# A gated recurrence with two expert stages: solve levels cut to the triangle's nonzero columns, own part's matmuls among level 3's

## The reference

```python
for t in range(S):
    y[:, :, t] = np.einsum('bhd,bhde->bhe', rt, state)
    Sa = np.einsum('bhde,bhe->bhd', state, at)
    state_decay = state * wt[:, :, None, :] - np.einsum('bhd,bhe->bhde', Sa, bt)
    state = state_decay + np.einsum('bhd,bhe->bhde', vt, kt)
```

## Time and profile before

| | |
|---|---|
| median of 3 runs | 992.5 us (991.58 to 993.65) |
| profiled execution | 993.9 us, span 992.2 us |
| TensorE busy | 947.2 us, 95% of the span |
| VectorE, ScalarE, GpSimd busy | 465.9, 270.5, 275.8 us |
| recurrence | about the first 385 us of the span |
| L956 (levels 2 and 3), L958 (level 4), L1028 (own) | 3072, 1536 and 1536 matmuls; 54.5, 18.1 and 20.7 us busy |

### The profile page before, as it was taken

How to read it: one execution, slowest core, us unless ns; L and a number is a source line. 1 busy time by engine, 2 the same in 40 slices (tenths; PEclk the granted TensorE clock), 3 DMA queues, 4 the chain that set the end, 5 groups by cost and what they waited for, 6 DMA issues and landing times.

```text
span 992.2 us, 51897 instructions
## 1 busy us (share of the span) xinstructions
PE 947.2 (95%) x23581; PEld 732.5 (74%) x23582; DVE 465.9 (47%) x964; ACT 270.5 (27%) x503; POOL 275.8 (28%) x297
## 2 busy tenths in 40 slices
PE   4689999999999999999999999999999999999995
PEld 3579989899898996454554554557888888888884
DVE  5447877887887762423143143162352322222220
ACT  1224444444444442201202202202212122122120
POOL 4535566556656651000011010010052101111111
PEclk9789999999999999999999999999999999999999
DMA  5216442333333321780100100047421111001000
GB/s 147 64 50 209 140 123 89 114 104 119 96 115 111 89 72 41 238 271 0 38 27 24 42 28 20 1 133 256 130 88 61 34 34 39 23 28 33 27 29 3
DMA packets 57704, 81.63 MB, mean 82 GB/s; under 512 B 22274, under 2 KB 37454, under 8 KB 57648
## 3 DMA queue, kind: packets, MB, share of 16 engines
q1 hardware_dynamic: 33536, 58.87, 19.0%
q10 hardware_dynamic: 21088, 13.32, 5.2%
q0 software_dynamic: 3024, 8.72, 2.4%
HBM read 68.04 MB, written 14.45 MB: 83 GB/s over the span
## 4 chain that ended last, share of the span: by engine, by line
PE 91%; issue 3%; DVE 2%; DMA 2%; POOL 1%; ACTq 0%; ACT 0%; POOLq 0%; SPq 0%; DVEq 0%
PE ps_D L1478 14%; PE ps_D L224 12%; PE ps_G L1460 6%; PE ps_E L1460 6%; PE ps_B L236 5%; PE ps_E L956 5%; PE ps_B L188 3%; PE ps_G L1467 3%; PE ps_D L1039 3%; PE ps_A L930 3%; PE ps_G L188 3%; PE ps_D L990 2%; PE ps_E L954 2%; PE ps_E L188 2%; PE ps_D L930 2%
## 5 line engine op out<-in xcount | busy, mean ns | idle before, releaser
L1478 PE MATMUL ps_D<-room,hT 128*128 x496 | 139.1, 433 | 0.8 <-issue 0.8
L224 PE MATMUL ps_D<-room 128*128 128x384 f32 x384 | 126.7, 489 | 0.6 <-DVE room L291 0.6
L1478 PEld LDWEIGHTS ps_D<-room,hT 128*128 128x128 f32 x496 | 91.8, 190 | 35.9 <-issue 1.3
L224 PEld LDWEIGHTS ps_D<-room 128*128 128x128 f32 x384 | 72.1, 190 | 51.5 <-issue 1.6
L1421 POOL DMA_INDIRECT out<-y,token x31 | 35.6, 1147 | 258.3 <-DVE y L1585 224.7
L550 POOL DMA_INDIRECT sorted_rows<-rows,slot x24 | 23.9, 997 | 278.3 <-DVE slot L542 272.2
L894 POOL TENSOR_TENSOR room<-room 32x256 f32<-32x256 f32 x96 | 69.5, 724 | 106.5 <-DVE room L1310 101.1
L1521 ACT ACTIVATE hT<-ps_G 128x512 f32<-128x512 f32 x31 | 18.5, 598 | 217.6 <-PE ps_E L1467 211.4
L1585 DVE TENSOR_SCALAR y<-ps_D,x_in 128x320 f32<-128x320 f32 x31 | 17.0, 550 | 125.9 <-PE ps_D L1478 117.5
L1568 DVE COPY w_own<-room 128x1024 f32 x62 | 44.9, 729 | 62.3 <-PE ps_G L1460 33.8
L291 DVE TENSOR_TENSOR room<-ps_D,room 128x384 f32<-128x384 f32 x32 | 17.8, 558 | 113.2 <-PE ps_D L224 107.8
(11 more groups left out here) (225 smaller groups left out, 1646.2 us busy)
## 6 DMA issues: line engine op xcount, KB each, us to landing
room<-in_moe_w SPq DMA_DIRECT2D x8, 1280.0 KB, 12.6
room<-in_moe_w SPq DMA_DIRECT2D x8, 1024.0 KB, 9.2
room<-in_kb SPq DMA_DIRECT2D x48, 160.0 KB
room<-in_vt SPq DMA_DIRECT2D x24, 320.0 KB, 3.1
x_in<-sorted_rows ACTq DMA_DIRECT2D x27, 161.0 KB, 2.3
room<-in_w SPq DMA_DIRECT2D x48, 82.7 KB
room<-in_a SPq DMA_DIRECT2D x48, 80.0 KB
room<-in_r SPq DMA_DIRECT2D x48, 80.0 KB
```

The source lines that it names most:

```text
L224: mm = pe.matmul(self.vs_bank[n % 2][:, 0:TH], self.v[:, s, d * P:(d + 1) * P], self.wspT[:, s, t * TH:(t + 1) * TH], start=(s == 0), stop ...
L1478: mm = pe.matmul(self.ps_y, side.hT[:, u % 2, f, :], self.weights.w2[:, bass.ds(e, 1), f, :], start=(f == 0), stop=(f == self.NF - 1))
```

## The change

- Levels 2, 3 and 4 take as moving operand only the columns from 4, 8 and 16 on (`NONZERO`), in both halves; so 56, 48 and 16 columns instead of 64, 64 and 32. Squares and sums copy and add these columns alone.
- The powers of levels 2 and 3 get a buffer each beside the sum (`powers`, with `sums` as its last part), whose columns below `NONZERO` are set to zero once, by two small memsets at the start.
- `solveT` gets its first 16 columns by a copy on ScalarE from the sum after level 3, for which `unknowns` has a new wait (`solve_d`).
- own_part is no longer a group of its own between level 2 and scores_r. Its 64 matmuls are issued one by one behind each of the 64 of level 3 (`level_and_own`).
- ScalarE does square 3 ahead of the drain of `own`, then the new copy.

```diff
--- before.py
+++ after.py
@@ -658,13 +658,14 @@
         eng.wait_ge(self.blank_tile, 16)
 
 
-ZEROED = 13
+ZEROED = 15
 CONSTANTS = 29
 CH = 32
 CHUNKS = SEQ // CH
 GROUPS = 16
 WCOLS = GROUPS * (CH + 1) + 1
 ROUNDS = 5
+NONZERO = (0, 0, 4, 8, 16)
 Counts = namedtuple("Counts", "fixed now after later now2 after4 after16 now32")
 
 
@@ -683,7 +684,9 @@
         kb_end = sb("kb_end", 8, 2, 2, CH)
         kb_next, kb_tok = sb("kb_next", 2, 8, 2, HALF), sb("kb_tok", 8, 2, HALF)
         xa, xf = sb("xa", 2, 4, 2, CH), sb("xf", 2, 4, 2, CH)
-        pw, qi, qs = sb("pw", 8, CH), sb("qi", 2, 8, CH), sb("qs", 2, 8, CH)
+        pw, qi = sb("pw", 8, CH), sb("qi", 2, 8, CH)
+        powers = sb("powers", ROUNDS - 1, 8, CH)
+        sums = powers[:, ROUNDS - 2]
         solveT = sb("solveT", 8, CH)
         own, rhs = sb("own", 4, 2, HD), sb("rhs", 4, 2, HD)
         vu, vu_d = sb("vu", 2, 4, 2, HALF), sb("vu_d", 8, 2, HALF)
@@ -721,7 +724,7 @@
         q_d = [sem(f"q{n}_drained") for n in range(ROUNDS - 1)]
         flip_d = [sem(f"flip{n}_drained") for n in range(ROUNDS - 1)]
         sum_d = [sem(f"sum{n}_drained") for n in range(ROUNDS)]
-        xa_d, xf_d, init_d = (sem(x) for x in ("xa_d", "xf_d", "init_d"))
+        xa_d, xf_d, init_d, solve_d = (sem(x) for x in ("xa_d", "xf_d", "init_d", "solve_d"))
         scan_f, scan_b, whole_d, inv_d = (sem(x) for x in ("scan_f", "scan_b", "whole_d", "inv_d"))
         grow_d, ae_d, kbe_d, faded_d = (sem(x) for x in ("grow_d", "a_end_d", "kb_end_d", "faded_d"))
         passed = sem("waits_passed")
@@ -934,7 +937,7 @@
                     pe.wait_ge(y_d, t.after)
                     turn(B, lambda m: faded[:, m].rearrange("p n e -> p (n e)"), fT_f)
 
-                def doubling(t, l):
+                def level(t, l, own=False):
                     if l == 0:
                         pe.wait_ge(xf_d, t.later)
                         if not t.fixed or t.after >= 1:
@@ -946,6 +949,7 @@
                         else:
                             pe.wait_ge(sum_d[l - 1], t.after)
                     pe.sem_inc(passed, 1)
+                    kept = slice(NONZERO[l], CH)
                     for j, n, mp, o in blocks():
                         q, i = quad(2 * mp + o), 2 * n + j
                         if l == 0:
@@ -953,14 +957,28 @@
                         elif l == 1:
                             mm = pe.matmul(E[q, :, i, :], pw[q, i, :], qi[q, :, i, :], start=True, stop=True)
                         elif l < ROUNDS - 1:
-                            mm = pe.matmul(E[q, :, i, :], pw[q, i, :], qs[q, :, i, :], start=True, stop=True)
+                            mm = pe.matmul(E[q, :, i, kept], pw[q, i, :], powers[q, l - 2:ROUNDS - 1:ROUNDS - l, i, kept],
+                                           start=True, stop=True)
                         else:
-                            mm = pe.matmul(E[q, 1, i, :], pw[q, i, :], qs[q, 1, i, :], start=True, stop=True)
+                            mm = pe.matmul(E[q, 1, i, kept], pw[q, i, :], sums[q, i, kept], start=True, stop=True)
+                        if own:
+                            k = quad(2 * mp + 1 - o)
+                            last = pe.matmul(G[q, i * HD:(i + 1) * HD], xa[k, o, n, j, :], v_tok[k, o, n, j, :],
+                                             start=True, stop=True)
                     mm.then_inc(round_f[l], 1)
+                    if own:
+                        last.then_inc(own_f, 1)
+
+                def level_and_own(t, l):
+                    pe.wait_ge(ld_v, t.after16)
+                    if not t.fixed or t.now >= 1:
+                        pe.wait_ge(own_d, t.now)
+                    level(t, l, own=True)
 
                 def unknowns(t):
                     pe.wait_ge(rhs_d, t.now)
                     pe.wait_ge(sum_d[4], t.now)
+                    pe.wait_ge(solve_d, t.now)
                     pe.sem_inc(passed, 1)
                     for j, n, mp, o in blocks():
                         q, i = quad(2 * mp + o), 2 * n + j
@@ -1017,17 +1035,6 @@
-
-                def own_part(t):
-                    pe.wait_ge(ld_v, t.after16)
-                    if not t.fixed or t.now >= 1:
-                        pe.wait_ge(own_d, t.now)
-                    pe.sem_inc(passed, 1)
-                    for j, n, mp, o in blocks():
-                        q, k, i = quad(2 * mp + o), quad(2 * mp + 1 - o), 2 * n + j
-                        mm = pe.matmul(G[q, i * HD:(i + 1) * HD], xa[k, o, n, j, :], v_tok[k, o, n, j, :],
-                                       start=True, stop=True)
-                    mm.then_inc(own_f, 1)
 
                 def scores_a(t):
                     pe.wait_ge(ae_d, t.later)
@@ -1049,38 +1056,36 @@
                 t = counts(-2)
                 turn_kb(t)
                 scores_a(t)
-                doubling(t, 0)
+                level(t, 0)
                 pe.wait_ge(fold_d, 1)
                 pe.wait_ge(s_zero, ZEROED)
                 t = counts(-1)
-                doubling(t, 1)
-                own_part(t)
-                doubling(t, 2)
+                level(t, 1)
+                level(t, 2)
                 turn_kb(t)
-                doubling(t, 3)
+                level_and_own(t, 3)
                 scores_a(t)
-                doubling(t, 4)
-                doubling(t, 0)
+                level(t, 4)
+                level(t, 0)
                 pe.sem_inc(rh_f, 1)
                 pe.sem_inc(fT_f, 1)
                 pe.wait_ge(kn_d, 2)
                 with pe.Fori(0, CHUNKS - 1) as c:
                     t = counts(c)
                     unknowns(t)
-                    doubling(t, 1)
+                    level(t, 1)
                     outputs_state(t)
                     growth(t)
                     turn_vu(t)
-                    doubling(t, 2)
-                    own_part(t)
+                    level(t, 2)
                     scores_r(t)
-                    doubling(t, 3)
+                    level_and_own(t, 3)
                     turn_kb(t)
                     scores_a(t)
-                    doubling(t, 4)
+                    level(t, 4)
                     outputs(t)
                     right_state(t)
-                    doubling(t, 0)
+                    level(t, 0)
                     turn_state(t)
                 t = counts(CHUNKS - 1)
                 unknowns(t)
@@ -1132,7 +1137,8 @@
                     return x.rearrange("p (a m) j e -> p a (m j e)", a=2)
 
                 def square(x, l):
-                    drain((qs if l else qi)[:, 0], E[:, 0], round_f[l], x + 1, q_d[l])
+                    kept = slice(NONZERO[l], CH)
+                    drain((powers[:, l - 1] if l else qi[:, 0])[:, :, kept], E[:, 0, :, kept], round_f[l], x + 1, q_d[l])
 
                 gated.load_out(act, woutT, wgl)
                 gated.copy_fold(act, G[:, :].rearrange("p (d n) -> p d n", n=P), folded, fold_d)
@@ -1162,10 +1168,13 @@
                         drain(turned(vu_d), D[:, :, :], vT_f, c + 1, vu_d_done)
                     if is_chunk(x):
                         square(x, 2)
+                        square(x, 3)
                         if c >= 0:
                             act.wait_ge(rhs_d, x)
                         drain(own.rearrange("p n j e -> p (n j e)"), G[:, 0:8 * HD], own_f, x + 1, own_d)
-                        square(x, 3)
+                        if c >= 0:
+                            act.wait_ge(uu_f, x)
+                        drain(solveT[:, :, 0:NONZERO[4]], sums[:, :, 0:NONZERO[4]], sum_d[3], x + 1, solve_d)
                     if y == CHUNKS:
                         act.sem_inc(kn_d, 1)
                     if is_chunk(y):
@@ -1221,7 +1230,8 @@
                 def flip(x, l):
                     dve.wait_ge(q_d[l], x + 1)
                     dve.transpose(pw.rearrange("p i t -> p (i t)"),
-                                  (qs if l else qi)[:, 0].rearrange("p i t -> p (i t)")).then_inc(flip_d[l], 1)
+                                  (powers[:, l - 1] if l else qi[:, 0]).rearrange("p i t -> p (i t)")
+                                  ).then_inc(flip_d[l], 1)
 
                 def summed(x, l):
                     dve.wait_ge(round_f[l], x + 1)
@@ -1229,13 +1239,17 @@
                         dve.wait_ge(init_d, 4 * x + 4)
                     else:
                         dve.wait_ge(sum_d[l - 1], x + 1)
-                    out = solveT[:, :, :] if l == ROUNDS - 1 else qs[:, 1]
-                    dve.tensor_tensor(out, E[:, 1], (qi if l == 1 else qs)[:, 1], ALU.add).then_inc(sum_d[l], 1)
+                    kept = slice(NONZERO[l], CH)
+                    old = qi[:, 1] if l == 1 else sums
+                    new = solveT if l == ROUNDS - 1 else sums
+                    dve.tensor_tensor(new[:, :, kept], E[:, 1, :, kept], old[:, :, kept], ALU.add).then_inc(sum_d[l], 1)
 
                 for c in steps:
                     x, y, f = c + 1, c + 2, c + 3
```

(2 more changed lines are left out.)

## The result

The changed kernel takes 998.7 us (median of 8 runs, 997.42 to 999.7); the kernel before, measured beside it, 992.5 (8 runs, 990.26 to 995.65). The ratio is 1.0059, 95% interval 1.0046 to 1.0073: slower by more than the 0.2% that can be told from no change. The profiled execution took 998.95 us, its span 997.2, against 993.9 and 992.2 before. The forecast was 995.2, range 990.2 to 1001.0, with "slower" as the likeliest sign. The sign and the mechanism came out; the size came out 3.5 us short. (Further down, one execution of e10, of 5043 us, and one of the kernel before measured beside it, of 1196, are left out of the ratios.)

The account below looks back on a forecast made before the run. Bound: the loop through GpSimd, VectorE and TensorE's level 3 to scores. 19 x (+0.20 - 0.03) = +3.2, -0.3 for v, -0.3 for the last two turns: +2.6; on the median 992.5 + 2.7 = 995.2 us, range 990.2 to 1001.

Parts of the forecast that it names:

- The bound: Recurrence period of 14.33 us set by a loop through GpSimd, VectorE and TensorE's level 3 to scores; TensorE alone needs 14.08.
- rival E: TensorE's work, not the loop through GpSimd, sets the period: every period falls by 0.54, 981 us; chance 0.12.
- Own taken out of its old place: Own's group leaving TensorE between level 2 and scores_r gains nothing: level 3 still waits for sum 2, TensorE idles about 1.0.
- Level 3 with own: TensorE's merged group, inside the loop: M, first weight load to next group's, goes from 1.05 to 1.25, +0.20 a period.
- Rival B: The 128 merged matmuls go no more than four at a time: M = 1.5, +8, 1000.5 us; chance 0.14.
- C: The merged stream keeps the burst's pace: M = 1.05, -1.5, 991.0 us; chance 0.17.
- D: Weight loads in the merged group serialise: M at least 1.79, +14, 1006.5 us; chance 0.04.
- Rival A: The forecast itself: the loop holds, M between 1.15 and 1.35, +1 to +4, own range 993.5 to 996.5; chance 0.49.
- rival F: ScalarE's new wait decides, the drain behind it ending over 1.2 late: +5.7, 998 us; chance 0.04.
- Narrower sum in the loop: Sum 2 on VectorE, with 224 elements, saves 0.03 a period.
- v: Own is needed 2 us later, so its wait for loads of v, 0.30 over the 19 periods, goes: -0.3.
- The last turns: The two turns without a scan: level 3 starts 0.35 sooner and takes 0.20 longer, 2 x -0.15 = -0.3.

Follow-up runs that it names:

- e10: e2 with one wait more on GpSimd, so that a_end begins only after the forward scan: 982.4 us, ratio 0.9906, three executions.
- e4: The changed kernel with GpSimd's product grow put ahead of its product kb_end: 991.4 us, ratio 0.9976, period 14.01.
- e9: The changed kernel with one wait more on GpSimd, so that a_end begins only after the forward scan: 987.7 us, ratio 0.9956.
- e11: The kernel before with one wait more on GpSimd, so that a_end begins only after the forward scan: 988.1 us, ratio 0.9957.
- e3: The kernel before with only own's matmuls moved among level 3's, all columns full, no ScalarE copy: 1003.6 us, ratio 1.0092.
- e2: The changed kernel with narrow columns kept and own back as a group between level 2 and scores_r: 988.6 us, ratio 0.9940.
- e1: The changed kernel with one TensorE instruction more, so that the waits for v and own's drain come before those for flip 2 and sum 2: 997.7 us.
- e8: The changed kernel with own's matmuls among level 2's instead of level 3's, waits apart as in e1: 1003.2 us, ratio 1.0104.

## Why the forecast was right, and where it was short

**The bound.** Right. The loop through GpSimd, VectorE and the stretch of TensorE from level 3 to the scores sets the period. TensorE lost 11 us of work and the kernel lost 6 (rival E, 981 us, fell); e4, which touches nothing on TensorE, gained 0.67 a period. But the forecast took the loop's steps as given. It took the "2.10" from the scan's start to the state update as the price of a scan, where 0.92 of it was GpSimd's a_end next to it (1.18 in e9); e11 takes that out of the kernel before and gains 4 us.

**Own taken out of its old place: nothing.** Right, with the idle in two places instead of one: 0.68 before level 3's matmuls and 0.28 before those of scores_r (0.76 and 0.41 by the weight loads), which now waits for ScalarE to drain vu. The forecast had costed scores_r's earlier start at nothing without saying for whom it would wait. In the changed kernel it is covered by the wait before level 3.

**Level 3 with own: M = 1.25.** Measured 1.30, at the upper end (1.31) of the forecast's bounds. The step failed in its reason for going below that end, that the slow start is paid once and more tiles spread the stream. 1.30 less 0.195 over 127 is 8.7 ns a pair, within 0.1 of the pace of level 4. It also failed in the sentence that the narrowing of level 3 is worth nothing inside the merged group: e3 against after shows 0.10. What the rows gave (a group of own pace stays near 8.8 ns) was right; the lowering was a guess, and cost 19 x 0.05 = 1 us. Rival B (1.5), C (1.05) and D (1.79) fell. Behind D stood a rule of the Trainium skill, "TensorE: Matmul & The Clock Gate", Part 3, that a weight load overlaps matmuls in flight only when the row group differs. The serial stream that the forecast drew from it is not what this trace shows: the merged group takes 1.30, the two groups one by one 0.74 and 0.83 (e2), 1.57 in all. The same Part also lets a load into a background weight buffer run ahead; which of the two holds for these tiles no run here tells.

**Waits.** This is the term that was missing. The forecast listed no cost for moving own's two waits to level 3, since both were met long before. They still had to be issued, and behind the late one: 0.15 a period (e1), 19 x 0.15 = 2.9 us. Most of the 3.5 us by which the forecast was short is this. Rival A's own range ended at 996.5; that 998.7 still lies in the stated range is owed to the room left for B and F, whose mechanisms did not occur, and is luck.

**Narrower sum in the loop: -0.03.** Right (0.35 for 0.38). **v: -0.3.** Right: the steady periods after are 14.65 to 14.70 throughout, where before had two of 14.46 and 14.50. **The last turns: -0.3.** The two from level 4 to level 4 take 28.02 (358.64 to 386.66) for 28.16, so -0.14; the forecast had 13.9 for each, they are 14.01. **ScalarE's copy: 0.** Right, and rival F fell; right_state never waits for it. **The first turns and the rest: 0.** The first turns 0.4 more, the later stages 1.6 less; neither was traced to a cause.

The sum again with what was measured: 19 periods x 0.35 = 6.65, less 0.3 for v and 0.1 for the last period, is 6.25 against the 6.2 seen between the fourth turn of xa and the last. That the medians lie 6.2 apart as well is partly chance: in the profiles the rest takes 1.2 back, and one of the two executions lies 1.4 above its median.

## What to carry to other kernels

Before freeing the engine that shows 95%, close the loop: add up the steps from one instruction back to itself, and ask of each edit whether it lies in that sum. Here work was taken from where TensorE had slack in the making and put where every 10 ns counted; the same narrow columns, with the work left in its place, gain 0.6%. When groups are merged, their waits are merged too: those met long ago belong ahead, in an instruction of their own, and those that come late (v in e8) hold up everything in the group. And of each step in the loop, compare its duration with the shortest of the same shape elsewhere in the trace, because a neighbour may be in it.

## What was not expected of the hardware

**VectorE's scan and GpSimd.** The same scan of 529 elements took 1.26 with GpSimd idle, 1.63 when begun 0.5 before GpSimd's instruction ended, and 2.19 when begun 0.03 after a GpSimd instruction of 1.09. In the second of these GpSimd's next instruction, begun during the scan, took 2.04 instead of 1.09. Each time the length fits one standing until the other is nearly or wholly through (after: a_end ends at 220.46, the scan 1.13 later; e4: kb_end ends at 215.61, the scan 1.12 later, then a_end 0.89 after the scan; alone they take 1.26 and 1.09). The Trainium skill, "SBUF — State Buffer", section "SBUF: two separate sides", describes the port pair shared by VectorE (with two inputs in SBUF, against a GpSimd instruction that reads SBUF) and GpSimd as an exclusive lock, held for the whole instruction by whichever starts first. The trace agrees, but for the 0.13 to 0.20 by which the second is through sooner than a start at the other's end would give. Of the places tried here the dearest for a GpSimd instruction is just ahead of VectorE's critical one, which is where the order of before and after puts a_end, since one event releases both.

**Small tiles.** 128 recorded pairs of weight load and matmul on 32x32 tiles went through in 1.30 (48 and 40 columns), 1.34 (56 and 40) and 1.40 (64 and 40), 64 pairs in 0.83 (48) and 1.05 (64).

**Packed waits.** An event instruction that waits for nothing, but stands behind a late one, costs TensorE 0.15 here.
